# Reordering sums and convolution steps, an early split of `w_out2`, new homes for buffers and narrower mean squares in a fused attention and two-FFN kernel

## The chip, the cores and the metric

The kernel runs on one core of a Trainium2 chip. The metric is the device time of one execution in microseconds (us); lower is better.

## The reference

Eight batches of 576 rows go through linear attention with an RMS norm, a gated feed-forward layer with a spatial product, and a second feed-forward layer with a convolution over the sequence. All of it is in fp32.

```python
kv = einsum('bhsd,bhse->bhde', k, v)              # 8 heads of 64
out = einsum('bhsd,bhde->bhse', q, kv)
x = out / sqrt(mean(out * out, -1) + 1e-6) * g_norm   # -> [8, 576, 512]
h = relu(x @ w_in)                                # 512 -> 1024
u, v = h[..., :512], h[..., 512:]
v_n = (v - mean(v)) / sqrt(var(v) + 1e-6)
gated = u * (w_spatial @ v_n + b_spatial)         # 576 x 576 over the sequence
x = gated @ w_out                                 # 512 -> 512
h = relu(x @ w_in2)                               # 512 -> 1024
c = conv_w[0] * h[s-1] + conv_w[1] * h[s] + conv_w[2] * h[s+1]
out = (h * sigmoid(c)) @ w_out2                   # 1024 -> 512
```

## The kernel before

**Splitting.** Every large product takes fp32 values as a high part (rounded to fp32r by a copy on ACT, functions ending in `_hi`) and a low part (value less high part, on DVE or POOL, functions ending in `_lo`). Three matmuls (`PASSES`) make one product.

**First phase.** `w_out @ w_in2` is multiplied out once at the start (`w_product`). Then `body(b, ahead)` runs for b = 0 to 7 on each engine: PE computes key-value product and attention of batch b+1 (`kv_product`, `o_product`, `square_sum`), the v half (`v_product`, five row tiles i) and u half (`u_product`) of the first layer, and `spatial_product`, four column tiles m. ACT evicts (`v_relu`, `u_relu`, `o_copy`), squares, and takes roots. DVE normalises (`v_stats`, `v_normalise`), inverts the RMS root (`mean_square`, `inverse_root`), scales x, splits, and multiplies by the gate (`gate`, L1045). SP stores the gated activations of a batch and four differences of them (`t_block`, L1092, into the tile `t_then_s`) to a DRAM scratch.

**Second phase.** `body2(b, ...)` runs for b = 0 to 7. The product with the combined weight uses seven products in place of eight for a 2x2 blocking (`PRODUCTS`, Strassen's form as Winograd ordered it), for each of four groups g: `in_product` on PE (L614), six matmuls of 288 columns for each of 28 products a batch. They go to PSUM bank n % 8. ACT copies product 0 of each group (`first_copy`, L905, into `x1`), and DVE makes seven sums from it and the banks (`add`, L1172): the 576 columns of two blocks of h, f = g and f = g + 4. Then for each of the eight blocks e, in `F_ORDER`: relu (ACT, L875), first tap (`tap1`, ACT, L881), two more taps (`tap0`, `tap2`, DVE, L1202 and L1208), sigmoid (ACT, L886), times h (`mul`, DVE, L1213), high part (`h_hi`, ACT, L897 or L899), low part (`h_lo`, DVE, L1218 and L1219). `rows_product` (PE, L622) takes block e of it against `wout2` into four banks, 12 matmuls of 512 columns per e. The last 64 rows of two batches share one more pass of 24 matmuls after each odd batch. In between, the operands of batch b+1 are loaded from the scratch and split (`operand_hi`, L862; `operand_lo`, L1121), seven each.

**What sets the order.** Each engine's order is written out by hand and runs strictly in turn; semaphores join them. In `body2` DVE's loop is

```python
                for e in range(FT + 2):
                    g = e + 1
                    if g < GROUPS: sums_a(b, g)
                    if e < FT: tap0(b, e)
                    if g < GROUPS: sums_b(b, g)
                    if e >= 2: h_lo(b, odd, e - 2)
                    if e < FT: tap2(b, e)
                    if g < GROUPS: sums_c(b, g)
                    if 0 <= e - 1 < FT: mul(b, e - 1)
                if ahead: operand_lo(b + 1, k) for the seven k
```

**Between the phases.** `w_out2` (2 MB) is loaded by SP after the spatial weights are split; its eight blocks are split at the end of the last `body` (ACT L869, POOL L385) into `wout2`, which lies over `w_in`. `x1` lies in `t_then_s`, so the first `first_copy` waits until the last differences are in DRAM (`s_To`). In the last `body`, DVE makes all operand low parts before `gate(3)`, and `in_product` n = 2 waits for that gate.

## Time and profile before

| | |
|---|---|
| three runs | 841.52 us median (839.79 to 842.79) |
| profiled execution | 841.8 us, span of the trace 840.0 us |
| granted TensorE clock | 0.992 of full speed |
| busy share of the span | PE 96%, PE weight load 84%, DVE 72%, ACT 50%, POOL 5% |
| chain that ended last | PE 71%, DVE 18%, ACT 4%, issue 4%, DMA 2% |
| stages by PE | up to 40.1: start and `w_product`; 40.1 to 416.8: first phase; 416.8 to 835.9: second phase |

Busy shares are means over stages; a PE row counts a matmul's whole passage, and matmuls overlap, so the pitch between starts is what a matmul costs. A body of the second phase is read from the start of its first L614 matmul to that of the next body.

### The profile page before, as it was taken

To read this page: it belongs to the slowest core of one execution; us is meant where nothing else is said; L and a number is where in the kernel's file an instruction comes from. 1 tells how busy PE (TensorE), PEld (TensorE's weight loads), DVE (VectorE), ACT (ScalarE), POOL (GpSimd) and SP (SyncE) were. 2 spreads that over 40 slices of the span, in tenths; PEclk is the share of its full clock that TensorE was granted. 3 is DMA by queue.
4 is the path that set the end of the run, shared out by engine and by line. 5 is a ranking of instruction groups with operands and counts; after the bars stand their busy time and mean duration, and the time that the engine had idled before them with its cause. 6 is when DMAs were issued, how large, how long until landed. Compare 5 with 4: busy or idle time off the path is not lost.

```text
span 840.0 us, 16008 instructions
## 1 busy us (share of the span) xinstructions
PE 802.4 (96%) x5910; PEld 704.0 (84%) x5910; DVE 607.5 (72%) x1254; ACT 418.3 (50%) x753; POOL 41.1 (5%) x44
## 2 busy tenths in 40 slices
PE   8998999999999999999969999999999999999998
PEld 7678899897979899898868897978879797796976
DVE  3876666757665766758869878597885978669782
ACT  4654352526343443524715648456473655646563
POOL 3342000000000000000140000000000000000000
PEclk9999999999999999999979999999999999999999
DMA  9862433426262533331322111121201212102101
GB/s 317 276 238 58 181 115 120 179 75 248 71 253 57 197 105 116 106 92 64 114 85 99 51 35 65 64 99 51 99 22 42 98 50 98 50 13 98 50 1 62
DMA packets 34009, 88.48 MB, mean 105 GB/s; under 512 B 2514, under 2 KB 8882, under 8 KB 30004
## 3 DMA queue, kind: packets, MB, share of 16 engines
q1 hardware_dynamic: 33828, 87.99, 31.0%
q8 instruction: 21, 0.34, 0.2%
q14 instruction: 16, 0.13, 0.1%
q10 hardware_dynamic: 144, 0.01, 0.0%
HBM read 61.92 MB, written 26.08 MB: 105 GB/s over the span
## 4 chain that ended last, share of the span: by engine, by line
PE 71%; DVE 18%; ACT 4%; issue 4%; DMA 2%; SPq 0%; DVEq 0%; ACTq 0%
PE ps L446 23%; PE ps L622 17%; PE ps L614 14%; PE ps L477 11%; DVE h_and_sums L1172 3%; DVE work L1213 3%; DVE work L1208 3%; PE ps L397 2%; DVE v_hg_split L1219 2%; PE ps L413 2%; ACT v_hg_split L897 2%; DMA kv_raw<-kv_rest_dram 1%; PE ps L547 1%; DVE t_then_s L1092 1%; PE ps L425 1%
## 5 line engine op out<-in xcount | busy, mean ns | idle before, releaser
L622 PE MATMUL ps<-w_in_split,v_hg_split 128*128 128x512 f32 x832 | 209.1, 398 | 14.7 <-DVE v_hg_split L1219 13.9
L622 PEld LDWEIGHTS ps<-w_in_split,v_hg_split 128*128 128x128 f32 x832 | 151.8, 188 | 66.0 <-DVE v_hg_split L1219 33.5
L446 PE MATMUL ps<-w_sp_split,v_hg_split 128*128 128x288 f32 x896 | 122.2, 297 | 2.8 <-DVE w_sp_split L1061 2.4
L446 PEld LDWEIGHTS ps<-w_sp_split,v_hg_split 128*128 128x128 f32 x896 | 120.8, 190 | 3.5 <-issue 2.6
L446 PE MATMUL ps<-x_operand_split,w_in_split 128*128 128x288 f32 x768 | 104.3, 296 | 1.5 <-ACT work L704 1.5
L446 PEld LDWEIGHTS ps<-x_operand_split,w_in_split 128*128 128x128 f32 x768 | 102.2, 188 | 3.6 <-ACT work L704 1.9
L477 PE MATMUL ps<-w_in_split,x_operand_split 128*128 128x512 f32 x384 | 93.5, 396 | 0.0
L477 PEld LDWEIGHTS ps<-w_in_split,x_operand_split 128*128 128x128 f32 x384 | 70.4, 188 | 20.9 <-issue 6.1
L1172 DVE TENSOR_TENSOR h_and_sums<-t_then_s,ps 128x288 f32<-128x288 f32 x64 | 28.0, 453 | 62.0 <-PE ps L614 41.5
L1172 DVE TENSOR_TENSOR h_and_sums<-h_and_sums,ps 128x288 f32<-128x288 f32 x160 | 66.2, 449 | 8.2 <-PE ps L614 7.4
L614 PE MATMUL ps<-x_operand_split,w_combined_more 128*128 128x288 f32 x384 | 62.3, 298 | 0.0
L1045 DVE TENSOR_TENSOR work<-ps,work 128x576 f32<-128x576 f32 x32 | 24.0, 753 | 48.5 <-PE ps L446 48.5
L875 ACT ACTIVATE h_and_sums<-h_and_sums 128x576 f32<-128x576 f32 x64 | 43.1, 674 | 28.3 <-DVE h_and_sums L1172 28.3
L614 PEld LDWEIGHTS ps<-x_operand_split,w_combined_more 128*128 128x128 f32 x384 | 55.9, 191 | 0.5
L886 ACT ACTIVATE work<-work 128x576 f32<-128x576 f32 x64 | 43.0, 672 | 19.7 <-DVE work L1208 19.7
L1208 DVE SCALAR_TENSOR_TENSOR work<-h_and_sums,const_cols,work 128x576 f32<-128x576 f32 x64 | 51.9, 811 | 0.0
L1202 DVE SCALAR_TENSOR_TENSOR work<-h_and_sums,const_cols,work 128x576 f32<-128x576 f32 x64 | 51.9, 811 | 0.0
L881 ACT ACTIVATE work<-h_and_sums,const_cols 128x576 f32<-128x576 f32 x64 | 49.8, 778 | 2.1
L1213 DVE TENSOR_TENSOR work<-h_and_sums,work 128x576 f32<-128x576 f32 x64 | 48.0, 750 | 0.0
L899 ACT ACTIVATE v_hg_split<-work 128x576 fp32r<-128x576 f32 x32 | 22.0, 687 | 49.9 <-DVE work L1213 49.9
L1012 DVE BATCH_NORM_STATS2 bn_stats<-work 128x6 f32<-128x512 f32 (+1 forms) x40 | 27.6, 691 | 24.7 <-ACT work L699 18.3
L685 ACT ACTIVATE x_operand_split<-o_x 128x576 fp32r<-128x576 f32 x32 | 22.0, 687 | 47.0 <-DVE o_x L995 44.0
(124 smaller groups left out, 1137.4 us busy)
## 6 DMA issues: line engine op xcount, KB each, us to landing
kv_raw<-kv_main_dram SPq DMA_DIRECT2D x8, 2048.0 KB, 9.7
q_raw<-q_T_dram SPq DMA_DIRECT2D x8, 1152.0 KB, 5.3
operand_scratch<-t_then_s SPq DMA_DIRECT2D x8, 1152.0 KB, 5.3
operand_raw<-operand_scratch SPq DMA_DIRECT2D x8, 1152.0 KB, 5.5
out_dram<-work SPq DMA_DIRECT2D x32, 256.0 KB, 2.2
sq_then_r<-r_scratch SPq DMA_DIRECT2D x14, 576.0 KB, 6.3
operand_scratch<-work SPq DMA_DIRECT2D x24, 288.0 KB, 2.6
operand_more_raw<-operand_scratch SPq DMA_DIRECT2D x8, 864.0 KB, 7.2
```

Of the source, the lines that this page charges most:

```text
L446: last = pe.matmul(pair[bank][:, c, :], st, mo[:, c * HALF:(c + 1) * HALF], start=(n == 0), stop=(n == len(steps) - 1))
L477: last = pe.matmul(dst, x, w, start=(n == 0), stop=(n == len(st) - 1))
L614: last = pe.matmul(PS[:, n % 8, 0:HALF], st, mo, start=(i == 0), stop=(i == len(steps) - 1))
L622: last = pe.matmul(PS[:, ROW_BANK[i], :], x, wout2[:, w, F_ORDER[e], :], start=(e == 0 and n == 0), stop=(e == FT - 1 and n == len(PASSES) ...
L875: act.activation(h_sb[f][:, 1:S + 1], h_sb[f][:, 1:S + 1], ACT.Relu).then_inc(s_hr, 1)
L881: act.activation(t_sb[e % 2], h_sb[f][:, 1:S + 1], ACT.Copy, scale=cols[:, FT + f:FT + f + 1]).then_inc(s_t0, 1)
L886: act.activation(p_sb[e % 2], t_sb[e % 2], ACT.Sigmoid).then_inc(s_sig, 1)
L1012: dve.bn_stats(stats[0:n, :], v_sb[i % 2][0:n, :]).then_inc(s_vst, 1)
L1172: dve.tensor_tensor(dst, x, PS[:, (g * NPROD + k) % 8, 0:HALF], ALU.add).then_inc(s_sum, 1)
L1202: dve.scalar_tensor_tensor(out=t, in0=h_sb[f][:, 0:S], scalar=cols[:, f:f + 1], in1=t, op0=ALU.mult, op1=ALU.add).then_inc(s_cv1, 1)
L1208: dve.scalar_tensor_tensor(out=t, in0=h_sb[f][:, 2:S + 2], scalar=cols[:, 2 * FT + f:2 * FT + f + 1], in1=t, op0=ALU.mult, op1=ALU.add).th ...
L1213: dve.tensor_tensor(p_sb[e % 2], h_sb[F_ORDER[e]][:, 1:S + 1], p_sb[e % 2], ALU.mult).then_inc(s_mul, 1)
```

## The change

1. **Order of products and sums.** `PRODUCTS` is permuted so that block f = g is complete after product 4 of a group; `F_ORDER` takes it first. Sums and convolution steps are written out one by one in `body2` on DVE and ACT. `operand_hi` and `operand_lo` 0 to 2 of the next batch move between the last two `h_hi` and `h_lo`.
2. **`w_out2`.** Loaded in two halves by ACT's own queue in the first-phase bodies 1 and 2 (now unrolled), split there by ACT and POOL, stored to a DRAM scratch from ACT's queue, and loaded in split form by SP after batch 7's u products, four DMAs of 1 MB.
3. **Homes.** `x1`, `t_sb[1]`, `p_sb` and `o_sb` get other places; the three waits for stores move from before the second phase to the first sigmoid and the first output copy. The last four differences go to DVE's first `body2`. In the last `body` low parts 5 and 6 come after `gate(3)`.
4. **Weights.** `A12` and `A22` keep their low part in place; one wait of ACT on DVE goes.
5. **Mean squares.** `head_select` has a column per head, so `square_sum` takes 128 rows at once: 16 matmuls in place of 32, and `ms`, `std`, `r0` have 144 columns in place of 288.

```diff
-PRODUCTS = [(A11, B11), (S2, T2), (A12, B21), (S3, T3), (S1, T1), (A22, T4), (S4, B22)]
+PRODUCTS = [(A11, B11), (S2, T2), (A12, B21), (S1, T1), (S4, B22), (S3, T3), (A22, T4)]
-F_ORDER = [4, 0, 5, 1, 6, 2, 7, 3]
+F_ORDER = [0, 4, 1, 5, 2, 6, 3, 7]
...
+        x1 = [WK[:, S:S + HALF], WK[:, 3328:3328 + HALF]]
-        x1 = [TB[:, M + i * HALF:M + (i + 1) * HALF] for i in (0, 1)]
-        ms, std, r0 = (sb(n, [P, CH, QS]) for n in ("ms", "std", "r0"))
+        ms, std, r0 = (sb(n, [P, QS]) for n in ("ms", "std", "r0"))
...
@ SP, behind load_operands(0)
+            sp.wait_ge(s_wo2_st, 2 * DMA)
+            for h in (0, 1):
+                for c, part in ((LO, 0), (HI, 1)):
+                    sp.dma_start(wout2[:, c, h * MT:(h + 1) * MT, :].bitcast(F32),
+                                 wo2_dram[h, :, part * MT * M:(part + 1) * MT * M].rearrange("p (f n) -> p f n", f=MT)).then_inc(s_wo2_ld, DMA)
             store_gated(B - 1)
...
@ PE, square_sum
-                        for c in range(CH):
-                            r = slice(c * D, (c + 1) * D)
-                            last = pe.matmul(PS[g * 32:(g + 1) * 32, SSQ_BANK + c, 0:QS], sel[r, m, :],
-                                             rB[r, m, g * QS:(g + 1) * QS], start=(m == 0), stop=(m == MT - 1))
+                        last = pe.matmul(PS[g * 32:(g + 1) * 32, SSQ_BANK, 0:QS], sel[:, m, :],
+                                         rB[:, m, g * QS:(g + 1) * QS], start=(m == 0), stop=(m == MT - 1))
...
@ ACT, body, at the end of row tile i
+                    if isinstance(b, int) and b in (1, 2):
+                        if i == 0:
+                            wo2_load(b - 1)
+                        else:
+                            wo2_split(b - 1, i - 1)
...
+            def wo2_split(h, f):
+                act.wait_ge(s_wo2_in, (h + 1) * DMA)
+                act.activation(wo2_hi[:, f, :], wo2_raw[:, f, :], ACT.Copy).then_inc(s_wo2_hi, 1)
...
@ ACT, body2
+                h_hi(b, odd, 5)
+                sigmoid(b, 7)
                 if ahead:
+                    operand_hi(b + 1, 0)
+                    operand_hi(b + 1, 1)
+                h_hi(b, odd, 6)
+                if ahead:
+                    operand_hi(b + 1, 2)
+                h_hi(b, odd, 7)
...
@ DVE, body2, groups 2 and 3 alike, then the rest
+                sum_u2_c11(b, 3)
+                mul(b, 1)
+                sum_u4(b, 3)
+                tap0(b, 3)
+                sum_c12(b, 3)
+                sum_u3(b, 3)
+                h_lo(b, odd, 1)
+                sum_c22(b, 3)
+                sum_c21(b, 3)
+                tap2(b, 3)
+
+                mul(b, 2)
+                for e in range(4, FT):
+                    tap0(b, e)
+                    h_lo(b, odd, e - 2)
+                    tap2(b, e)
+                    mul(b, e - 1)
                 if ahead:
+                    operand_lo(b + 1, 0)
+                h_lo(b, odd, FT - 2)
+                mul(b, FT - 1)
+                if ahead:
+                    operand_lo(b + 1, 1)
+                    operand_lo(b + 1, 2)
+                h_lo(b, odd, FT - 1)
```

**ACT, end of the first `body2`.** Sigmoids are L886 before and L915 now, high parts of h L899 and L926, operand high parts L862 and L891, output copies L925 and L988. Before:

```order
L886 ACTIVATE work<-work 128x576
L899 ACTIVATE v_hg_split<-work 128x576
L886 ACTIVATE work<-work 128x576
L899 ACTIVATE v_hg_split<-work 128x576
L862 ACTIVATE x_operand_split<-operand_raw 128x576 x4
L862 ACTIVATE operand_more_split<-operand_more_raw 128x576 x3
L925 ACTIVATE work<-ps 128x512 x4
```

Now:

```order
L926 ACTIVATE v_hg_split<-work 128x576
L915 ACTIVATE work<-work 128x576
L891 ACTIVATE x_operand_split<-operand_raw 128x576 x2
L926 ACTIVATE v_hg_split<-work 128x576
L891 ACTIVATE x_operand_split<-operand_raw 128x576
L926 ACTIVATE v_hg_split<-work 128x576
L891 ACTIVATE operand_more_split<-operand_more_raw 128x576 x2
```

Two operand splits stand ahead of the seventh high part of h, a third ahead of the eighth.

**DVE, end of the first `body2`, now.** L1278 and L1284 are taps, L1289 `mul`, L1294 and L1295 `h_lo`, L1193 `operand_lo`; before, all seven operand splits stood behind the last `h_lo`.

```order
L1284 SCALAR_TENSOR_TENSOR work<-h_and_sums,const_cols,work 128x576
L1289 TENSOR_TENSOR work<-h_and_sums,work 128x576
L1193 TENSOR_TENSOR x_operand_split<-operand_raw,x_operand_split 128x576
L1294 TENSOR_TENSOR rest_split<-work,v_hg_split 128x64
L1295 TENSOR_TENSOR v_hg_split<-work,v_hg_split 128x512
L1289 TENSOR_TENSOR work<-h_and_sums,work 128x576
L1193 TENSOR_TENSOR x_operand_split<-operand_raw,x_operand_split 128x576 x2
L1294 TENSOR_TENSOR rest_split<-work,v_hg_split 128x64
L1295 TENSOR_TENSOR v_hg_split<-work,v_hg_split 128x512
```

One low part of an operand now stands ahead of the seventh `h_lo`, two more ahead of the eighth.

**ACT, first-phase `body` 1, row tiles 0 to 2, now** (with the semaphores waited on). L704 is `v_relu`, L719 `v_hi`, L714 `v_root`, L675 and L680 `o_copy` and `square`:

```order
L680 ACTIVATE sq_then_r<-o_x 128x576 [waits s_xm,s_oc]
L792 DMA w_out_raw<-w_out_dram 128x4x512 [waits s_b,s_sp_lo]
L704 ACTIVATE work<-ps 128x512 [waits s_vlo,s_v]
L719 ACTIVATE v_hg_split<-work 128x512 [waits s_vn]
L714 ACTIVATE vsd<-ve 128x1 [waits s_ve]
L796 ACTIVATE v_hg_split<-w_out_raw 128x512 [waits s_wo2_in]
L704 ACTIVATE work<-ps 128x512 [waits s_vlo,s_v]
L675 ACTIVATE o_x<-ps 128x576 [waits s_xr,s_o]
```

L792 and L796 are new; the third `v_relu` and all that follows it stand behind L796's wait for the load that L792 issued three instructions earlier.

## Rows read from the trace of the kernel before

**Rows 1.** What PE waited for: line, releaser, us in total, times, longest

```profile
PE ps L622 <- DVE v_hg_split L1219: 13.9, 16, 1.1
PE ps L614 <- DVE work L1045: 5.0, 1, 5.0
PE ps L614 <- ACT t_then_s L905: 4.3, 1, 4.3
PE ps L446 <- DVE w_sp_split L1061: 2.4, 1, 2.4
```

**Rows 2.** Timeline of PE: start, length, instructions, idle before; second-phase bodies 0, 1, 2

```profile
416.84 0.96 PE L614 MATMUL ps<-x_operand_split,w_combined_more 128*128 128x288 f32 x6
...
477.66 0.95 PE L614 MATMUL ps<-x_operand_split,w_combined_more 128*128 128x288 f32 x6
...
530.67 0.61 PE L622 MATMUL ps<-w_in_split,v_hg_split 128*128 128x512 f32 x2
...
531.36 0.95 PE L614 MATMUL ps<-x_operand_split,w_combined_more 128*128 128x288 f32 x6
...
558.62 20.64 PE L622 MATMUL ps<-w_in_split,v_hg_split 128*128 128x512 f32 x84 [0.72 <-DVE v_hg_split L1219]
579.10 0.95 PE L614 MATMUL ps<-x_operand_split,w_combined_more 128*128 128x288 f32 x6
```

**Rows 3.** Timeline of DVE in second-phase body 2

```profile
551.48 0.82 DVE L1172 TENSOR_TENSOR h_and_sums<-t_then_s,ps 128x288 f32<-128x288 f32 x2 [1.79 <-ACT t_then_s L905]
...
559.21 0.75 DVE L1213 TENSOR_TENSOR work<-h_and_sums,work 128x576 f32<-128x576 f32 x1
...
572.78 0.69 DVE L1219 TENSOR_TENSOR v_hg_split<-work,v_hg_split 128x512 fp32r<-128x512 f32 x1
...
575.02 0.69 DVE L1219 TENSOR_TENSOR v_hg_split<-work,v_hg_split 128x512 fp32r<-128x512 f32 x1
575.63 2.76 DVE L1121 TENSOR_TENSOR x_operand_split<-operand_raw,x_operand_split 128x576 fp32r<-128x576 f32 x4
```

**Rows 4.** Timeline of ACT in second-phase body 2

```profile
574.76 2.39 ACT L862 ACTIVATE x_operand_split<-operand_raw 128x576 fp32r<-128x576 f32 x4
```

**Rows 5.** Costliest groups: count, busy us, mean ns of one, idle before

```profile
L1172 DVE TENSOR_TENSOR h_and_sums<-h_and_sums,ps 128x288 f32<-128x288 f32 x160 | 66.2, 449 | 8.2 <-PE ps L614 7.4
...
L1208 DVE SCALAR_TENSOR_TENSOR work<-h_and_sums,const_cols,work 128x576 f32<-128x576 f32 x64 | 51.9, 811 | 0.0
```

**Rows 6.** Timeline of DVE between the phases

```profile
417.49 5.32 DVE L1121 TENSOR_TENSOR operand_more_split<-operand_more_raw,operand_more_split 128x576 fp32r<-128x576 f32 x3
```

**Rows 7.** Timeline of POOL, the eight low parts of `w_out2`

```profile
415.65 13.55 POOL L385 TENSOR_TENSOR w_in_split<-w_out_raw,w_in_split 128x512 fp32r<-128x512 f32 x8 [345.79 <-ACT w_in_split L869]
```

**Rows 8.** Timeline of ACT in first-phase body 1

```profile
100.44 0.69 ACT L675 ACTIVATE sq_then_r<-o_x 128x576 f32<-128x576 f32 x1
...
104.57 0.60 ACT L699 ACTIVATE work<-ps 128x512 f32<-128x512 f32 x1 [0.69 <-PE ps L477]
```

**Rows 9.** DMA issues: count, KB each, median us from issue to landing

```profile
q_raw<-q_T_dram SPq DMA_DIRECT2D x8, 1152.0 KB, 5.3
```

**Rows 10.** Stretches: us, busy by engine, PE clock, DMA share, GB/s

```profile
102.00:104.00 2.00, 2.00 (x11) 1.65 (x10) 1.45 (x5) 1.17 (x3) 0.00 (x0) 1.00 1.01 410
```

**Rows 11.** Timeline of DVE in the inverse root, bodies 0 and 1

```profile
68.61 1.57 DVE L980 TENSOR_TENSOR std<-std,ms 128x288 f32<-128x288 f32 x1
...
116.00 1.95 DVE L976 RECIPROCAL r<-std 128x288 f32<-128x288 f32 x1 [0.61 <-ACT std L679]
...
118.48 0.46 DVE L980 TENSOR_TENSOR std<-std,ms 128x288 f32<-128x288 f32 x1
```

**Rows 12.** Timeline of PE, first-phase bodies 3 and 4: square sums, key-value products

```profile
204.46 1.24 PE L425 MATMUL ps<-sq_then_r,head_select 64*32 64x144 f32 x64
205.63 12.99 PE L446 MATMUL ps<-x_operand_split,w_in_split 128*128 128x288 f32 x96
...
233.40 2.55 PE L397 MATMUL ps<-kv_raw 128*64 128x64 f32 x80
```

More of the change, by code:

```diff
@@ L297, in _ @@
                 store_gated(b)
-            sp.wait_ge(s_sp_lo, NT)
-            sp.wait_ge(s_b, 1)
-            sp.dma_start(wo2_raw[:, :, :], w_out2.rearrange("(f p) n -> p f n", p=P)).then_inc(s_wo2_in, DMA)
             spread_r(B - 1)
@@ L757, in body @@
                     u_relu(b, 3)
+                    if isinstance(b, int) and b in (1, 2):
+                        wo2_store(b - 1)
                     for m in range(MT):
@@ L852, in _ @@
             body(0, True)
-            with act.Fori(1, B - 1) as b:
+            body(1, True)
+            body(2, True)
+            with act.Fori(3, B - 1) as b:
                 body(b, True)
@@ L885, in sigmoid @@
                 act.wait_ge(s_hlo, b * FT + max(e - 1, 0))
+                if e == 0 and isinstance(b, int) and b == 0:
+                    for s in s_go:
+                        act.wait_ge(s, DMA * B)
+                    act.wait_ge(s_T, 4 * B)
+                    act.wait_ge(s_wo2_st, 2 * DMA)
                 act.activation(p_sb[e % 2], t_sb[e % 2], ACT.Sigmoid).then_inc(s_sig, 1)
@@ L924, in body2 @@
                     act.wait_ge(s_od[i], DMA * b)
+                    if i == 0 and isinstance(b, int) and b == 0:
+                        act.wait_ge(s_To, DMA * B)
                     act.activation(o_sb[i], PS[:, ROW_BANK[i], :], ACT.Copy).then_inc(s_oev, 1)
@@ L937, in _ @@
             act.wait_ge(s_pad, 1)
-            for s in s_go:
-                act.wait_ge(s, DMA * B)
-            act.wait_ge(s_To, DMA * B)
             run(0, False)
@@ L1221, in body2 @@
             def body2(b, odd, ahead):
-                sums_a(b, 0)
-                sums_b(b, 0)
-                sums_c(b, 0)
-                for e in range(FT + 2):
-                    g = e + 1
-                    if g < GROUPS:
-                        sums_a(b, g)
-                    if e < FT:
-                        tap0(b, e)
-                    if g < GROUPS:
-                        sums_b(b, g)
-                    if e >= 2:
-                        h_lo(b, odd, e - 2)
-                    if e < FT:
-                        tap2(b, e)
-                    if g < GROUPS:
-                        sums_c(b, g)
-                    if 0 <= e - 1 < FT:
-                        mul(b, e - 1)
@@ L1241, in body2 @@
-                if ahead:
-                    for k in range(NPROD):
+                first = isinstance(b, int) and b == 0
+                sum_u2_c11(b, 0)
+                if first:
+                    t_a(B - 1)
+                sum_u4(b, 0)
+                sum_c12(b, 0)
+                if first:
+                    t_b(B - 1)
+                sum_u3(b, 0)
+                if first:
+                    t_c(B - 1)
+                sum_c22(b, 0)
+                sum_c21(b, 0)
+                sum_u2_c11(b, 1)
@@ new lines, in body2 @@
+                tap0(b, 0)
+                sum_u4(b, 1)
+                tap2(b, 0)
+                sum_c12(b, 1)
+                sum_u3(b, 1)
+                tap0(b, 1)
+                sum_c22(b, 1)
+                sum_c21(b, 1)
+                tap2(b, 1)
+                sum_u2_c11(b, 2)
+                mul(b, 0)
+                sum_u4(b, 2)
+                tap0(b, 2)
+                sum_c12(b, 2)
+                sum_u3(b, 2)
+                h_lo(b, odd, 0)
+                sum_c22(b, 2)
@@ new lines, in body2 @@
+                sum_c21(b, 2)
+                tap2(b, 2)
+                sum_u2_c11(b, 3)
[14 more added lines that the diff above has]
+                    mul(b, e - 1)
@@ L1243, in body2 @@
+                if ahead:
+                    operand_lo(b + 1, 0)
+                h_lo(b, odd, FT - 2)
+                mul(b, FT - 1)
+                if ahead:
+                    operand_lo(b + 1, 1)
+                    operand_lo(b + 1, 2)
+                h_lo(b, odd, FT - 1)
+                if ahead:
+                    for k in range(3, NPROD):
                         operand_lo(b + 1, k)
```

194 lines of the change are left out of this document (119 added, 75 removed).

## The prediction

> **What bounds the kernel now.** I read the page first: PE is busy 96% of a span of 840.0 us, so only two things can help, less work for PE or fewer of its waits. The waits of PE come next [rows 1]: the largest sum is rows_product waiting for h_lo, two long waits in each second-phase body; then one stop of 5.0 on a gate and one of 4.3 on first_copy, both between the phases; then 2.4 in first-phase body 0. In the timeline of PE [rows 2] second-phase body 2 lasts 579.10 - 531.36 = 47.74 us and body 1, which has the 24 matmuls for rest rows, 531.36 - 477.66 = 53.70. Body 0 lasts 477.66 - 416.84 = 60.82, 13 more than body 2.
>
> What ends body 2 is seen by joining rows of PE and DVE. The 84 matmuls of e = 1 to 7 take 579.10 - 558.62 = 20.48, 0.244 each, where three in a row without a wait go from 530.67 to 531.36, 0.23 each. The seventh h_lo ends at 572.78 + 0.69 = 573.47 [rows 3], 42.11 after the body's start; PE has 24 matmuls left from there and ends 5.63 later. The last h_lo, 575.71, is 3.39 before the end and does not set it. So a second-phase body is as long as DVE and ACT need to bring the seventh h_lo, plus 5.6.
>
> In the first phase the 2.4 in body 0 is the only stop of PE over 1 us that this view has once the bodies run; from body 1 on PE is the bound.
>
> **Part 1: order in body2, bodies 1 to 6.** Up to mul(2), DVE executes exactly the same instructions in both orders: 28 sums, four of each DVE tap, mul and h_lo of e = 0 and 1. Only its waits differ. Before, mul(2) starts at 559.21, 27.85 after the start [rows 3], and the longest wait on the way is 1.79 on ACT's first_copy for group 3. In the new order I walk the same span: group 0 goes with PE and ends 6.2 after the start; 1.2 and 0.4 waiting for the copy and the third product of group 1; 21 sums, eight taps, two mul and two h_lo in a row, 0.37, 0.73, 0.66 and 0.74 apiece, which is a row's duration less 0.08 or so ([rows 5], and mul and h_lo in [rows 3]), since neighbours overlap as the four splits in 2.76 do, 16.3; and now two waits of the 1.79 kind, since the copies of groups 2 and 3 both stand behind a sigmoid that needs the tap just finished, 1.8 and 1.7. Sum 27.7: the same.
>
> From there both orders repeat tap0, h_lo, tap2, mul at one pace, but a relu now stands ahead of the third h_hi on ACT, +0.3. The tail differs more. Two operand splits stand on ACT ahead of the seventh h_hi. Four in a row take 2.39 [rows 4], 0.57 apart, so h_hi(6) comes 1.1 later and h_lo(6) ends 43.5 after the start where it was 42.1. Behind it DVE has mul, two low parts of 0.67 and h_lo(7), which ends at 46.2; 12 matmuls are left there, 2.8. Both ways give 49.1, against 47.74: **+1.35** for each of bodies 1 to 6, which is +8.1. Body 7 has no operands to split: +0.3. The bounds are what rows allow for the two causes: at least 0 if PE's backlog hides the tail, at most +2.0 if both of ACT's terms and a further 0.6 of the low parts fall on the path. So 0 to +12 for the six.
>
> **Part 2: between the phases.** PE reaches the first in_product at 416.84 as before. Before, DVE made seven low parts ahead of gate(3), three of them in 5.32 [rows 6] beside POOL's splits at 415.65 to 429.20 [rows 7]; PE stood 5.0, then 4.3 for the stores in front of x1, and ran slowly behind both. Now POOL is silent here, low parts 5 and 6 come behind the gate, and x1 needs no store. gate(3) is made when the last spatial product ends, about 417.1, done at 417.8; in_product 2 wants it at 418.4. The four differences now stand in DVE's group 0 and move it back by 1.5 net. So body 0 lasts 49.1 + 1.5 = 50.6 against 60.8: **-10.2**. The seven operand splits hide under spatial products. The first sigmoid now carries the waits for stores. SP issues 4 MB of w_out2 ahead of them at about 402; with 2 MB of operands at 410 GB/s [rows 10] that is done by 420, the stores by 424, and the sigmoid comes at 429. The low bound is that nothing but the two stops goes, -9.3 and -3 of slow matmuls at most, -12; the high bound -8, if ACT or DVE is late by two more.
>
> **Part 3: w_out2 in bodies 1 and 2.** ACT issues 1 MB at the end of row tile 0, 101.1, just behind a square [rows 8]. The first split stands ahead of the third v_relu, which ran at 104.57, and behind that come the copies and squares for which PE's last v_product waits. A lone load of 1152 KB takes 5.3 [rows 9], and here the DMA engines are full with SP's loads of keys, values and queries (410 GB/s, share 1.0 [rows 10]). Sharing alike, 1 MB needs 2.5 to start plus 5.2 at half of 410: it lands about 109. ACT stops for 5, the third v_relu goes from 104.6 to 109.6, the fourth square from 108 to 113.5, and PE, which wanted it at 110.2, loses 3.3. The fourth and fifth v_relu lose more behind three further splits, and POOL's four low parts hold DVE. The shorter inverse root, 1.9 less, gives back the end of that chain. I take **+4.0** a body, +8. Bounds: +1.5 each if the load lands in the 5.3 of [rows 9], +5.5 if it lands at 111: 3 to 11 for both.
>
> While POOL split the spatial weights in body 0, one instruction of the inverse root took 1.57 where it takes 0.46 [rows 11]. By the Trainium skill (SBUF — State Buffer, Who interferes with whom) a DVE instruction with two SBUF inputs is blocked for the whole of a GpSimd instruction that reads SBUF. By that rule, the trace agrees. I count about 1 a body for POOL inside the 4.0, since ACT is the later one for most of it; the whole of it is a rival below.
>
> **Part 4: mean squares.** The reciprocal took 1.95 and three products 0.46 for 288 columns [rows 11]; at half the columns about 1.9 goes from each body, hidden where PE has no gap. In body 0 it is on the path of the 2.4 stop [rows 1], of which 1.9 goes, and part of the slow matmuls behind it: **-3**, bounds -1 to -4. At the start PE is busy with w_product until the root is needed: 0. On PE the square sum takes 205.63 - 204.46 = 1.17 a batch [rows 12] and eight tiles side by side become four with half the matmuls, so I take 0; bounds: half of it gone, -4.7 for all, or twice as long, +9. Key-value products use all 128 rows in two column tiles, and 80 of them pass in 2.5, 0.031 each.
>
> The Trainium skill (TensorE: Matmul & The Clock Gate, The mechanism under Packing small matmuls) says that a weight load overlaps running matmuls only when its row group differs. With all 128 rows no load would be hidden, and the square sum would grow; how far is worked out as a rival below. By that rule, the 0.031 for full-row tiles speaks against it.
>
> **Part 5: the rest.** Weights in place take 2.4 of waits off DVE in the last body; it is inside part 2. Four more memsets lie under the first DMA. Stores of w_out2 from ACT's queue, 2 MB each, come where DMA is idle: 0.
>
> **Sum.** 840.0 + 8.1 + 0.3 - 10.2 + 8.0 - 3.0 = 843.2 in span, +1.8 around it as in the profiled 841.8: 845.0. The median shown is 0.3 below that execution, so **844.6**.
>
> **Rivals.**
> *The tail costs nothing* (0.20). PE's backlog at e = 6 is larger than I think, or the operand halves fit the gaps that DVE had anyway. Then part 1 is +0.3 a body, 844.6 - 6.3 = 838.3, faster than before. For it: 2.24 lie between the last two h_lo [rows 3] where mul and h_lo take 1.4, so 0.8 was free. Against: ACT's two splits stand in front of h_hi(6), not beside it. It decides at an h_lo(6) that ends before 42.5.
> *The load is quick* (0.15): 1.5 a body in part 3, 839.6. For it: descriptors of two queues may not share alike. Against: share 1.0.
> *The body falls to PE's own work* (0.07): 168 matmuls at 12.99/96 = 0.135 [rows 12] and 96 at 0.23 [rows 2], 44.8, which is -2.9 a body. In seven bodies, in place of +8.4: 844.6 - 8.4 - 20.3 = 815.9. For it: DVE has two blocks ready when the products end. Against: its pace per block behind that is unchanged.
> *The first sigmoid waits* (0.11), slower. SP's 6 MB go at two thirds of 410 GB/s, end near 427, the 2 MB of stores behind them near 434; the sigmoid wants them at 429, and DVE's mul and PE follow it, +5: 850. It decides from 429 on.
> *POOL's splits fall on the path whole* (0.05), eight of 13.55/8 = 1.69 [rows 7], +13.5 in place of +8: 850.1. The rule above gives this one. *The square sum doubles* (0.03), +1.17 in each of eight batches: 854.0, the other rule's.
> *The change does not free the stop between the phases* (0.04), another wait takes its place: 854.8.
>
> **Numbers.** The forecast has 0.35. A measurement tells 0.3%, 2.5 us, from no change: 839.0 to 844.0. Faster: the tail, PE's own work, some of the quick load and of the forecast's lower end, 0.32. Slower: the last four rivals and six tenths of the forecast, 0.44. The rest 0.24. The range holds the forecast with its bounds (837 to 851 alone), the tail and the quick load together (833) and the late sigmoid: 833 to 851.
>
> **What would show it.** Right: second-phase bodies of 49 and 55 us by the start of L614; body 0 near 50.6 with no stop of PE before in_product 9; in bodies 1 and 2 a wait of ACT for DMA of 4 to 5, and a first-phase body near 51; body 0 three shorter. Wrong: second-phase bodies below 47.7, L425 rows longer than 1.2, no wait of ACT on w_out_raw, or a wait of the first sigmoid for the scratch.

## The result, and the profile after

The changed kernel takes 856.67 us (median of 4, 855.42 to 857.69) against 841.39 us (839.79 to 842.79) for the kernel before beside it: 1.0182 times the time, 95% interval 1.0158 to 1.0205. Slower was forecast, with 0.44, but by 3; it is 15.3, outside the range. The profiled execution has a span of 853.6 against 840.0, at the same granted clock of 0.992.

First the waits of PE in the changed kernel (us in total, times, longest), to be held against [rows 1]:

```profile
PE ps L627 <- DVE v_hg_split L1295: 17.4, 18, 1.3
PE ps L482 <- ACT work L704: 10.5, 2, 7.4
PE ps L627 <- DVE h_and_sums L1244: 5.5, 7, 1.1
...
PE ps L404 <- DMA kv_raw<-kv_rest_dram: 2.6, 1, 2.6
PE ps L430 <- DVE sq_then_r L1022: 1.7, 1, 1.7
PE ps L451 <- DVE w_sp_split L1121: 1.3, 1, 1.3
```

The stops of 5.0 and 4.3 between the phases are gone. New in second place is `v_product` waiting for ACT's `v_relu` (L704), 10.5 in two waits, and this is in the bodies that carry `w_out2`. The timeline of PE gives the bodies their lengths. First phase, bodies 0 to 2 (start, length, instructions, idle before):

```profile
58.53 1.19 PE L430 MATMUL ps<-sq_then_r,head_select 128*32 128x144 f32 x32
...
74.84 15.08 PE L451 MATMUL ps<-w_sp_split,v_hg_split 128*128 128x288 f32 x112 [1.28 <-DVE w_sp_split L1121]
...
113.61 3.83 PE L482 MATMUL ps<-w_in_split,rest_split 128*128 128x512 f32 x8 [7.41 <-ACT work L704]
...
147.62 2.55 PE L404 MATMUL ps<-kv_raw 128*64 128x64 f32 x80
...
167.12 2.29 PE L482 MATMUL ps<-w_in_split,rest_split 128*128 128x512 f32 x7 [3.10 <-ACT work L704]
```

Second phase, the starts of bodies 0, 1, 2 and 3, with the stops inside body 2; [rows 2] are their counterpart:

```profile
431.83 0.96 PE L619 MATMUL ps<-x_operand_split,w_combined_more 128*128 128x288 f32 x6
...
482.62 0.95 PE L619 MATMUL ps<-x_operand_split,w_combined_more 128*128 128x288 f32 x6
...
537.58 0.95 PE L619 MATMUL ps<-x_operand_split,w_combined_more 128*128 128x288 f32 x6
...
560.93 6.17 PE L627 MATMUL ps<-w_in_split,v_hg_split 128*128 128x512 f32 x24 [0.80 <-DVE h_and_sums L1244]
568.27 11.95 PE L627 MATMUL ps<-w_in_split,v_hg_split 128*128 128x512 f32 x48 [1.17 <-DVE v_hg_split L1295]
581.23 5.76 PE L627 MATMUL ps<-w_in_split,v_hg_split 128*128 128x512 f32 x24 [1.01 <-DVE v_hg_split L1295]
586.83 0.96 PE L619 MATMUL ps<-x_operand_split,w_combined_more 128*128 128x288 f32 x6
```

Body by body, each the difference of two such starts (before's are from its own timeline, read alike):

| us | before | forecast | after | difference |
|---|---|---|---|---|
| first phase, body 0 | 52.1 | 49.1 | 49.4 | -2.7 |
| body 1 | 47.1 | 51.1 | 57.8 | +10.7 |
| body 2 | 47.1 | 51.1 | 54.2 | +7.1 |
| second phase, body 0 | 60.8 | 50.6 | 50.8 | -10.0 |
| bodies 1 to 6, each | 53.7, 47.7 | 55.0, 49.1 | 55.0, 49.25 | +1.3 to +1.5 |

With six of the last kind (+8.4), 0.3 more in the start, 0.2 more in the last body and 0.5 less in the first phase's other five, that is 13.6, the whole difference of the spans. (The profiled execution took 855.4, 1.2 under its median, and that of the kernel before 841.8, 0.4 over its own: that is the way from 13.6 to 15.3.) All lines but two are within 0.3 of the forecast. First-phase bodies 1 and 2 cost 17.8 where 8 stood.

What ACT did there (timeline of ACT, then the DMA issues between 94 and 116 us: count, KB each, us from issue to landing):

```profile
98.13 0.39 ACTq L792 DMA_DIRECT2D w_out_raw<-w_out_dram  x1
...
101.27 0.20 ACT L714 ACTIVATE vsd<-ve 128x1 f32<-128x1 f32 x1 [0.71 <-DVE ve L1077]
112.45 0.63 ACT L796 ACTIVATE v_hg_split<-w_out_raw 128x512 fp32r<-128x512 f32 x1 [10.97 <-DMA w_out_raw<-w_out_dram]
112.98 0.58 ACT L704 ACTIVATE work<-ps 128x512 f32<-128x512 f32 x1
```
```profile
kv_raw<-kv_main_dram SPq DMA_DIRECT2D x1, 2048.0 KB, 11.6
...
q_raw<-q_T_dram SPq DMA_DIRECT2D x1, 1152.0 KB, 8.6
w_out_raw<-w_out_dram ACTq DMA_DIRECT2D x1, 1024.0 KB, 14.3
kv_raw<-kv_rest_dram SPq DMA_DIRECT2D x1, 256.0 KB, 12.9
```

ACT stood for 11.0 in front of the first split, with the third `v_relu` behind it. The load took 14.3 to land. SP had issued the store of 1.2 MB of differences at 93.94 and 2.4 MB of keys and values at 94.91 and 95.77; `w_out2` came behind them at 98.13, and 1.2 MB of queries at 103.45. By issue time plus landing the keys and values were in at 106.5 and 108.7, the queries at 112.1 and `w_out2` last, at 112.4. In body 2 the order was another: issued at 155.90, `w_out2` landed at 165.9, the queries only at 168.7. For body 1 the stretches say the same (us, busy of PE, PEld, DVE, ACT and POOL, PE clock, DMA share, GB/s):

```profile
104.00:106.00 2.00, 2.00 (x10) 1.49 (x8) 0.00 (x0) 0.00 (x0) 0.00 (x0) 1.00 1.03 320
106.00:108.00 2.00, 0.20 (x1) 0.00 (x0) 0.00 (x0) 0.00 (x0) 0.00 (x0) 1.00 1.08 356
108.00:110.00 2.00, 0.00 (x0) 0.00 (x0) 0.00 (x0) 0.00 (x0) 0.00 (x0) 1.00 1.04 432
110.00:112.00 2.00, 0.00 (x0) 0.00 (x0) 0.00 (x0) 0.00 (x0) 0.00 (x0) 0.60 0.27 111
112.00:114.00 2.00, 0.39 (x1) 0.39 (x2) 0.41 (x1) 1.55 (x3) 0.85 (x1) 0.50 0.00 0
```

The DMA engines are full until 110, from 106.2 no compute engine works, and then PE's clock falls to 0.5, the lower of its two levels (1.2 and 2.4 GHz). So the eight matmuls behind the stop take 3.83.

### The profile page after: what moved, and what is told of

Its sections match the earlier page's. It is cut to its first block and busy times, and to the rows that moved or that the text cites. A ratio compares the mean times of both kernels' runs of the same rounds, so it can differ in the third digit from the quotient of the medians.

```text
span 853.6 us, 15487 instructions
## 1 busy us (share of the span) xinstructions
PE 802.4 (94%) x5654; PEld 700.6 (82%) x5654; DVE 588.0 (69%) x1254; ACT 419.3 (49%) x753; POOL 40.1 (5%) x48
## 5 line engine op out<-in xcount | busy, mean ns | idle before, releaser
L451 PE MATMUL ps<-w_sp_split,v_hg_split 128*128 128x288 f32 x896 | 120.4, 295 | 1.7 <-DVE w_sp_split L1121 1.3
L915 ACT ACTIVATE work<-work 128x576 f32<-128x576 f32 x64 | 44.0, 687 | 94.0 <-DVE work L1284 94.0
L1244 DVE TENSOR_TENSOR h_and_sums<-work,ps 128x288 f32<-128x288 f32 x64 | 27.5, 453 | 71.7 <-PE ps L619 39.4
L1105 DVE TENSOR_TENSOR work<-ps,work 128x576 f32<-128x576 f32 x32 | 24.1, 755 | 61.2 <-PE ps L451 61.0
L899 ACT ACTIVATE h_and_sums<-h_and_sums 128x576 f32<-128x576 f32 x64 | 43.1, 674 | 27.9 <-DVE h_and_sums L1244 27.7
L1278 DVE SCALAR_TENSOR_TENSOR work<-h_and_sums,const_cols,work 128x576 f32<-128x576 f32 x64 | 51.9, 811 | 0.0
L1284 DVE SCALAR_TENSOR_TENSOR work<-h_and_sums,const_cols,work 128x576 f32<-128x576 f32 x64 | 51.9, 811 | 0.0
L905 ACT ACTIVATE work<-h_and_sums,const_cols 128x576 f32<-128x576 f32 x64 | 49.1, 767 | 0.5
L1289 DVE TENSOR_TENSOR work<-h_and_sums,work 128x576 f32<-128x576 f32 x64 | 48.1, 751 | 0.0
L1295 DVE TENSOR_TENSOR v_hg_split<-work,v_hg_split 128x512 fp32r<-128x512 f32 x64 | 43.8, 684 | 0.0
## 6 DMA issues: line engine op xcount, KB each, us to landing
w_out_split_scratch<-v_hg_split ACTq DMA_DIRECT2D x2, 2048.0 KB, 10.5
```

The lines of the kernel that those rows point to most:

```text
L451: last = pe.matmul(pair[bank][:, c, :], st, mo[:, c * HALF:(c + 1) * HALF], start=(n == 0), stop=(n == len(steps) - 1))
L899: act.activation(h_sb[f][:, 1:S + 1], h_sb[f][:, 1:S + 1], ACT.Relu).then_inc(s_hr, 1)
L905: act.activation(t_sb[e % 2], h_sb[f][:, 1:S + 1], ACT.Copy, scale=cols[:, FT + f:FT + f + 1]).then_inc(s_t0, 1)
L915: act.activation(p_sb[e % 2], t_sb[e % 2], ACT.Sigmoid).then_inc(s_sig, 1)
L1244: dve.tensor_tensor(dst, x, PS[:, (g * NPROD + k) % 8, 0:HALF], ALU.add).then_inc(s_sum, 1)
L1278: dve.scalar_tensor_tensor(out=t, in0=h_sb[f][:, 0:S], scalar=cols[:, f:f + 1], in1=t, op0=ALU.mult, op1=ALU.add).then_inc(s_cv1, 1)
```

## The experiments

Two theories for bodies 1 and 2: ACT's stand for the load is the cost (1), or the added work itself, four splits on ACT, POOL's hold on DVE and 1 MB more of DMA, is (2). And for the second phase: which part of the new order costs the 1.35 a body, and whether it gives anything. All times are medians beside runs of the kernel before on the same chip (841.52, 841.80 and 841.93 in the three sets). PE's first wait for keys and values, near 16 us, takes 0.9 to 2.6 in different executions, so that spans scatter by over 1 us; body lengths do not, and are compared below.

| run | time | ratio to before (95%) | bodies 1, 2 | body 0 of second phase | odd, even body |
|---|---|---|---|---|---|
| before | 841.5 | | 47.1, 47.1 | 60.8 | 53.7, 47.7 |
| changed | 856.7 | 1.018 (1.016 to 1.021) | 57.8, 54.2 | 50.8 | 55.0, 49.25 |
| e1 split late | 837.2 | 0.995 (0.994 to 0.997) | 47.0, 47.1 | 50.9 | 55.0, 49.25 |
| e2 load early | 838.4 | 0.996 (0.995 to 0.998) | 47.6, 47.6 | 50.8 | 55.0, 49.3 |
| e3 old tail | 847.6 | 1.007 (1.005 to 1.010) | 57.7, 53.6 | 49.7 | 53.9, 48.2 |
| e4 rows of 8 KB | 850.6 | 1.011 (1.009 to 1.013) | 54.8, 53.0 | 50.8 | 55.0, 49.3 |
| e5 mean squares alone | 838.1 | 0.996 (0.994 to 0.997) | 47.0, 47.0 | 60.9 | 53.7, 47.7 |
| e6 low parts first | 854.6 | 1.015 (1.013 to 1.017) | 57.7, 54.8 | 50.0 | 55.0, 49.3 |
| e7 copies first | 828.1 | 0.984 (0.981 to 0.986) | 57.7, 54.3 | 47.3 | 51.8, 45.9 |
| e8 = e1 + e7 | 810.7 | 0.963 (0.961 to 0.965) | 47.0, 47.1 | 47.3 | 51.8, 45.9 |
| e10 = e1 + e3 + e6 + e7 | 802.2 | 0.954 (0.951 to 0.957) | 47.0, 47.2 | 45.4 | 50.7, 44.8 |
| e11 before, copy first | 833.6 | 0.991 (0.988 to 0.993) | 47.1, 47.1 | 61.3 | 52.8, 46.8 |

### e1: the splits of w_out2 at the end of the body

```diff
-                    if isinstance(b, int) and b in (1, 2):
-                        if i == 0:
-                            wo2_load(b - 1)
-                        else:
-                            wo2_split(b - 1, i - 1)
+                    if isinstance(b, int) and b in (1, 2) and i == 0:
+                        wo2_load(b - 1)
...
-                    if isinstance(b, int) and b in (1, 2):
-                        wo2_store(b - 1)
                     for m in range(MT):
                         x_hi(b + 1, m)
+                    if isinstance(b, int) and b in (1, 2):
+                        for f in range(MT):
+                            wo2_split(b - 1, f)
+                        wo2_store(b - 1)
```

> The changed kernel with its load of w_out2 where it is (after row tile 0 of bodies 1 and 2), but with ACT's four splits and the store moved behind the four x_hi at the body's end, when the load has long landed. Bodies 1 and 2 last 57.8 and 54.2 in the changed kernel, 47.05 without w_out2. Theory 1 (the cost is ACT standing for the load, 11.0 and 6.6, with PE starved and slow behind it): both bodies at 47.1 to 48.5, the span shorter by 15 to 18, time about 840. Theory 2 (the cost is the work itself: four splits on ACT, four low parts on POOL that hold DVE, 1 MB beside the other loads): the work is all still there, so at least half of the 17.8 stays, both bodies 50 to 53, time 848 to 854.

Measured: 837.16, 19.5 less than the changed kernel. Bodies 1 and 2 take 47.0 and 47.1 where they took 57.8 and 54.2, 17.8 less: all that the two bodies had cost. The same load, eight splits, POOL's eight low parts and the two stores are still there. In e1's timeline ACT does the four splits in one piece, without a wait, and the eight matmuls that took 3.83 take half of that:

```profile
105.11 1.97 PE L482 MATMUL ps<-w_in_split,rest_split 128*128 128x512 f32 x8
```
```profile
129.54 2.18 ACT L795 ACTIVATE v_hg_split<-w_out_raw 128x512 fp32r<-128x512 f32 x4
```

The load lands no sooner here: the median of the two is 15.8, longer than the 12.2 in the changed kernel. Nobody waits for it. Theory 2 falls.

### e2: the loads a body earlier

```diff
-                        if i == 0:
-                            wo2_load(b - 1)
-                        else:
+                        if i:
                             wo2_split(b - 1, i - 1)
...
                     for m in range(MT):
                         x_hi(b + 1, m)
+                    if isinstance(b, int) and b in (0, 1):
+                        wo2_load(b)
```

> The changed kernel with the splits where they are, between the row tiles, but each load issued a body earlier: behind the four x_hi of bodies 0 and 1 (the second waits there for the store of the first half). Theory 1: the load has landed by the first split, so the stop of 11.0 and 6.6 is gone; left are four splits of 0.6 in ACT's chain and POOL's low parts, both bodies 47.5 to 49.5, time 841 to 844. Theory 2: the splits in the chain and POOL's hold on DVE are the cost: both bodies 51 or more, time 849 or more. If ACT's wait for the store at the end of body 1 holds up its keys and values copy for body 2, body 2 alone stays long by some us.

Measured: 838.35, bodies 1 and 2 both 47.6. The splits are in the middle of ACT's chain, as in the changed kernel, but do not wait (timeline of ACT, load and first split of body 1; DMA issues):

```profile
84.11 0.39 ACTq L792 DMA_DIRECT2D w_out_raw<-w_out_dram  x1
...
101.55 0.62 ACT L796 ACTIVATE v_hg_split<-w_out_raw 128x512 fp32r<-128x512 f32 x1
```
```profile
w_out_raw<-w_out_dram ACTq DMA_DIRECT2D x2, 1024.0 KB, 5.7
```

Issued where SP's large loads are not under way, the same 1 MB lands in 5.7. Splits and POOL's share together cost 0.6 a body; the prediction's 4.0 had held 1 for POOL alone.

### e4: larger pieces for the same load

The host lays `w_out2` out as `[2, 128, 4 * 512]`, so that a partition reads 8 KB in one piece and not four rows of 2 KB. Nothing else differs.

> The changed kernel with w_out2 laid out in DRAM so that each partition's part of a half is 8 KB in one piece instead of four rows of 2 KB. In the changed kernel the two loads land 14.3 and 10.0 after their issue. If the load is slow because its packets are small, it lands in 8 or less and bodies 1 and 2 are shorter by 8 or more. If it is slow because the DMA engines are full with SP's loads of keys, values and queries (share 1.0 until 110) and share in some other way than alike, landing stays at 10 to 14 and the time within 2.

Measured: 850.56, between the two expectations. In body 1 the load lands 10.7 after its issue in place of 14.3, in body 2 9.5 in place of 10.0, and the bodies are 3.0 and 1.2 shorter. The queues between 94 and 116 us, first of the changed kernel, then of e4 (packets, MB, share of 16 engines; q10 is ACT's queue, q1 SP's):

```profile
q1 hardware_dynamic: 1088, 4.72, 57.9%
q10 hardware_dynamic: 528, 1.05, 15.0%
```
```profile
q1 hardware_dynamic: 1058, 4.65, 58.7%
q10 hardware_dynamic: 144, 1.05, 11.5%
```

In body 1, 1.05 MB in 14.3 us are 73 GB/s, a fifth of the 360 or so that moved; in e4 98 GB/s, a quarter. In body 2 it is 105 GB/s, and 110 in e4. So the size of a piece has some part in the share (2.0 KB a packet against 4.3 KB in SP's queue), but even with 7.3 KB ACT's load did not get half. By the Trainium skill (DMA: Bandwidth & Descriptors, Queues, rings and completion order) a DMA engine takes the queues that have work in turn, a packet at a time. The runs agree in so far as larger pieces got more in body 1. The page's packet holds several descriptors, though, while the rows above count 512 packets of 2 KB or 128 of 8 KB and 16 others for one load, so that no share follows from the rule here. What sets the fifth stays open.

### e3: operand splits behind the last h_hi and h_lo

```diff
                 sigmoid(b, 7)
-                if ahead:
-                    operand_hi(b + 1, 0)
-                    operand_hi(b + 1, 1)
                 h_hi(b, odd, 6)
-                if ahead:
-                    operand_hi(b + 1, 2)
                 h_hi(b, odd, 7)
                 if ahead:
-                    for k in range(3, NPROD):
+                    for k in range(NPROD):
                         operand_hi(b + 1, k)
```
DVE's `operand_lo` likewise, behind `h_lo(7)`.

> The changed kernel with the seven operand splits of bodies of the second phase all behind h_hi(7) on ACT and h_lo(7) on DVE, as before the change. Theory 1 (two operand splits ahead of h_hi(6) make h_lo(6) late by 1.1 to 1.4, which sets when the last 24 matmuls of out_product start): an even body 49.25 becomes 48.1, all seven bodies together 7 to 8 shorter, time about 849. Theory 2 (the rest of the order, two waits of 1.8 and 1.7 for the first copies of groups 2 and 3, sets the end alone, and the tail is hidden): no change, within 2. Theory 3: with all splits at the end, the next body's products wait for operands 0 to 2: PE stops up to 1.5 at each start and the time is the same or longer.

Measured: 847.63. Each of the seven bodies with operands ahead is 1.03 to 1.14 shorter, 7.5 in all; the rest of the 9.0 lies ahead of the second phase, in the scatter and bodies 1 and 2. So 1.1 of the 1.3 to 1.5 that each of bodies 1 to 6 lost is the tail, by the path that the prediction gave: two operand splits on ACT in front of h_hi(6).

### e7: the first copies ahead of the sigmoids

```diff
                 h_relu(b, 2)
+                first_copy(b, 2)
                 sigmoid(b, 1)
                 tap1(b, 2)
-                first_copy(b, 2)
...
+                first_copy(b, 3)
                 sigmoid(b, 2)
                 h_relu(b, 4)
-                first_copy(b, 3)
```

> The changed kernel with ACT's first_copy(2) ahead of sigmoid(1) and first_copy(3) ahead of sigmoid(2), in each body of the second phase. DVE's two waits of 1.80 and 1.71 for these copies go. Theory 1 (these waits stand on the chain to h_lo(6), which starts the last 24 matmuls): h_lo(6) ends up to 3.5 earlier, PE's stops of 1.2 and 1.0 in out_product go, and an even body 49.25 falls to what PE itself needs, 22.4 + 6.2 + 12.0 + 5.8 = 46.3; time 834 to 840. Theory 2 (DVE only waits elsewhere, since each sum waits for its product anyway, and the tail of operand splits sets the end): below 1 a body, time 850 or more.

Measured: 828.14, 28.5 less than the changed kernel and 13.4 less than the kernel before, from two moved lines. In the changed kernel DVE stood in front of the sums of groups 2 and 3 in each body (timeline of DVE, body 2):

```profile
552.76 0.82 DVE L1244 TENSOR_TENSOR h_and_sums<-work,ps 128x288 f32<-128x288 f32 x2 [1.80 <-ACT work L932]
...
559.98 0.82 DVE L1244 TENSOR_TENSOR h_and_sums<-work,ps 128x288 f32<-128x288 f32 x2 [1.71 <-ACT work L932]
```

ACT's `first_copy` (L932) stood behind a sigmoid, and the sigmoid needs the tap that DVE makes just ahead of these sums: each engine waited for the other in turn. With the copies first both waits are gone, and all eight bodies are 3.1 to 3.5 shorter: nearly all of the two waits was on the path. PE's stops in body 2 fall to one:

```profile
552.95 16.87 PE L627 MATMUL ps<-w_in_split,v_hg_split 128*128 128x512 f32 x72
570.84 5.75 PE L627 MATMUL ps<-w_in_split,v_hg_split 128*128 128x512 f32 x24 [1.01 <-DVE v_hg_split L1295]
```

### e5: the mean squares in the kernel before

The fifth part of the change alone, in the kernel before: `sel`, `selT`, `square_sum`, `ms`, `std` and `r0` as the change has them.

> The kernel before with one part of the change alone: mean squares in 144 columns (one tile of four mean squares by two halves instead of two, and half as wide ms, std and r). Theory 1: the inverse root is 1.9 shorter and only body 0 has a stop that it ends (2.41), so body 0 goes from 52.1 to 49.4 as in the changed kernel, and all else stays: 2.7 less, time 838.7. Theory 2: body 0 of the changed kernel is shorter for another reason: no change. On PE the square sums stay at 1.12 to 1.2 a batch; twice that would cost 9.

Measured: 838.11, 3.7 less than before. Body 0 of the first phase takes 49.4 as in the changed kernel, 2.7 less; no other body moves by over 0.1, and the rest lies ahead of body 0, in the scatter. Of the 2.7, 1.1 is the shorter stop and 1.5 that 112 matmuls behind it run at full pace:

```profile
73.80 15.09 PE L444 MATMUL ps<-w_sp_split,v_hg_split 128*128 128x288 f32 x112 [1.26 <-DVE w_sp_split L1059]
```

Before, they took 16.61 behind a stop of 2.4. But e11 below, which changes nothing in the first phase, has the same stop and full pace behind it (before, then e11):

```profile
75.66 16.61 PE L446 MATMUL ps<-w_sp_split,v_hg_split 128*128 128x288 f32 x112 [2.41 <-DVE w_sp_split L1061]
```
```profile
75.10 15.09 PE L446 MATMUL ps<-w_sp_split,v_hg_split 128*128 128x288 f32 x112 [2.40 <-DVE w_sp_split L1063]
```

The granted clock from 76 to 80 us was 0.61 and 0.54 before and 1.00 in e11. So the stop of 2.4 is followed by slow matmuls in some executions and not in others. The 1.1 is shown; that the narrower mean squares also saved the 1.5 is not. The median of e5 is 3.7 lower and its times lie closer together (838.0 to 838.9, before 839.9 to 843.6), which fits slow stretches that have become rare, but one trace each doesn't prove it.

### e6: low parts 5 and 6 ahead of the gate again

```diff
-                    operand_lo(0, 3)
-                    operand_lo(0, 4)
+                    for k in range(3, NPROD):
+                        operand_lo(0, k)
                 gate(b, 3)
...
-                else:
-                    operand_lo(0, 5)
-                    operand_lo(0, 6)
```

> The changed kernel with low parts 5 and 6 of the first operands ahead of gate(3) again in the last body of the first phase, as before the change; the splits of w_out2 stay in bodies 1 and 2. The kernel before had stops of 5.0 and 4.3 there. Theory 1 (POOL's splits, which slowed three low parts to 5.32, made the stop): the low parts take 0.7 apiece, gate(3) is at most 1.4 later than now, time within 1.5. Theory 2 (the order alone, low parts ahead of the gate): in_product stops for 3 or more again, time 3 or more longer.

Measured: 854.64, and body 0 of the second phase 50.0 in place of 50.8. No stop came back. In the timeline of DVE the low parts end as `gate(3)` (L1105) can start, at 431.95 here (432.10 in the changed kernel):

```profile
429.14 1.42 DVE L1190 TENSOR_TENSOR operand_more_split<-operand_more_raw,operand_more_split 128x576 fp32r<-128x576 f32 x2
430.48 0.75 DVE L1190 TENSOR_TENSOR x_operand_split<-operand_raw,x_operand_split 128x576 fp32r<-128x576 f32 x1
431.14 0.75 DVE L1190 TENSOR_TENSOR operand_more_split<-operand_more_raw,operand_more_split 128x576 fp32r<-128x576 f32 x1
431.95 0.76 DVE L1105 TENSOR_TENSOR work<-ps,work 128x576 f32<-128x576 f32 x1
```

So the order of low parts and gate alone makes no stop, and moving two low parts behind the gate, into DVE's way at the first sums, cost 0.8. What is left for the stop of 5.0 are two things, and no run takes them apart. Beside POOL's splits three low parts took 5.32 [rows 6], and with the one ahead of them (second line below, before) these four took 6.6, where they take 2.8 here: 3.8 of the 5.0. And DVE came to them later: its third gate (first line) stood 1.3 ahead of the first `in_product` [rows 2] and stands 3.2 ahead of it in e6, since two waits for ACT's high parts of the weights, 1.2 each, are gone.

```profile
415.55 0.75 DVE L1045 TENSOR_TENSOR work<-ps,work 128x576 f32<-128x576 f32 x1
416.22 1.35 DVE L1121 TENSOR_TENSOR x_operand_split<-operand_raw,x_operand_split 128x576 fp32r<-128x576 f32 x1
```

By these figures moving `w_out2` out of this place was the larger part. The other stop, 4.3 for the stores in front of `x1`, is gone in the changed kernel, but no run undoes its part alone.

### e8, e10 and e11: together, and the copy alone in the kernel before

e8 is e1 with e7. e10 adds e3 and e6. e11 is the kernel before with `first_copy(3)` ahead of `h_hi(0)` and `sigmoid(1)`, and nothing else.

> The changed kernel with the splits of w_out2 at the end of bodies 1 and 2 and the first copies of groups 2 and 3 ahead of the sigmoids, both. If both theories hold and act in different places, the gains add: 16 to 18 in bodies 1 and 2 and 17 to 22 in the second phase, time 818 to 824, below the kernel before (841.4). If one of them fails, 835 to 842.

> Four edits to the changed kernel together: splits of w_out2 at the end of bodies 1 and 2, the first copies of groups 2 and 3 ahead of the sigmoids, all operand splits behind the last h_hi and h_lo, low parts 3 to 6 ahead of gate(3). The first two together gave 810.7 with an even body of the second phase of 45.9 and one stop of 1.0 to 1.1 left in each, ahead of the last matmuls, where h_lo(6) comes late behind an operand split. Theory 1 (that stop is the tail's): it goes, even bodies fall to 45.0 and odd ones to 50.9, 6 less, and low parts first give 0.8: time 803 to 806. Theory 2 (the tail is now hidden and splits at the end make the next body's first products wait): 808 to 813.

> The kernel before with one edit: the first copy of group 3 ahead of h_hi(0) and sigmoid(1) on ACT in each body of the second phase; nothing of the change. DVE waited 1.79 for that copy, PE stopped 1.0 and 0.7 behind. Theory 1 (the copy behind a sigmoid is what keeps a body above PE's own work, in either order, and the alternation of sums and steps is itself worth nothing): an even body 47.7 falls to about 46.0, all eight 12 to 14 less, time 828 to 830. Theory 2 (only the new order, with its earlier sums, can use the early copy): less than 4 gained, time 838 or more.

Measured: e8 810.68, 7 below its range; the two gains add. Apart they gave 19.5 and 28.5, together 46.0, and the bodies have the same lengths as alone. The range had been added up from smaller gains. e10 802.23, 0.954 of the kernel before (0.951 to 0.957), faster than both kernels: 39.7 less than before in its own set. PE no longer stops in an even body at all:

```profile
532.34 22.57 PE L627 MATMUL ps<-w_in_split,v_hg_split 128*128 128x512 f32 x96
554.76 0.96 PE L619 MATMUL ps<-x_operand_split,w_combined_more 128*128 128x288 f32 x6
```

That body lasts 44.81: 28 products at 0.80 and 96 matmuls at 0.234, PE's own work.

e11 lies between its theories: 833.64, an even body 46.8 and not 46.0. The bodies of the second phase give 6.1 of its 8.2 in span; 1.5 is the full pace in first-phase body 0, which its edit doesn't touch. The wait of 1.79 went, but PE still stops once and takes the other 84 matmuls in 20.47 from start to start, 0.244 each as before [rows 2], not 0.234:

```profile
551.48 3.00 PE L622 MATMUL ps<-w_in_split,v_hg_split 128*128 128x512 f32 x12
555.18 20.63 PE L622 MATMUL ps<-w_in_split,v_hg_split 128*128 128x512 f32 x84 [0.70 <-DVE v_hg_split L1221]
```

It goes at DVE's pace: `h_lo` starts come 2.98 apart there, and 12 matmuls need 2.8. So the new order of sums and steps is worth something: with copies early and the tail as before in both, 46.8 in the old order against 44.8 in the new, 2.0 a body. With two waits for copies and operand splits in the tail it became a loss of 1.3 to 1.5.

## Why the prediction was wrong

**Part 1, right.** An even body was forecast at 49.1 and takes 49.25, an odd one 55.0 and takes 55.0. The steps hold too: `mul(2)` starts at 565.40, 27.8 after the start (forecast 27.7); DVE waits 1.80 and 1.71 for the copies (1.8 and 1.7); h_lo(6) ends 43.6 after the start (43.5). e3 gives the tail 1.08 and leaves 0.4 for the rest (1.1 and 0.3 forecast). What the text didn't do is ask what the body would be without the two waits that it had worked out. e7 brings it to 45.9 and e10 to 44.8, the figure of the rival *the body falls to PE's own work*.

**Part 2, right.** 50.8 against 50.6, no stop at the start, and a stop of 1.1 at the sums that the four differences delay. Of the causes that it named, low parts 5 and 6 behind the gate were not needed: e6 shows 0.8 the other way. POOL's splits, argued from [rows 6] and [rows 7], fit 3.8 of the stop of 5.0, and the 2.4 of waits for weights of part 5 fit the rest; e6 leaves only these two, and no run undoes either alone. The first sigmoid did not wait for the stores; that rival falls.

**Part 3, the step that failed.** "Sharing alike, 1 MB needs 2.5 to start plus 5.2 at half of 410: it lands about 109." That is 7.9 after its issue; it was 14.3 in body 1 and 10.0 in body 2, and ACT stood 11.0 and 6.7, not 5. In body 1 the load got a fifth of the traffic and not half, and came through with the last of SP's. All of it together, 5.8 MB with the store ahead, ends at 108 by the 410 of [rows 10], which is 9.9 after the issue (98.1 in this trace, 101.1 in the prediction's time) and so the prediction's own high bound. By the 348 that the stretches from 94 to 110 show in the mean, known only afterwards, it ends at 110.5. The second omission is the clock. In body 1 the 10.7 is 8.5 of stops (3.3 forecast) and 1.9 of eight matmuls at half pace. In body 2, where the load landed at that high bound (+5.5), it costs 7.1: 3.9 of stops, nearly as forecast, and 3.2 of slow matmuls, square sums and u products behind them (13.97 for 96 of these in place of 12.98), with a granted clock of 0.50 to 0.69 from 168 to 176 us. About 5 of the 17.8 are thus PE running slowly, for which the prediction had no term. And what it did count, splits and POOL's hold, costs 0.6 a body (e2), or nothing at the body's end (e1).

The rule of the Trainium skill (SBUF — State Buffer, Who interferes with whom) holds in the records. Beside a subtraction on POOL of 1.28 one product of the inverse root takes 0.93 where 0.31 is usual, and a small operation 0.83 for 0.16:

```profile
120.18 0.83 DVE L1090 TENSOR_TENSOR vrs<-vr,vrf 128x1 f32<-128x1 f32 x1 [0.19 <-DVE vrf L1088]
...
125.92 0.93 DVE L1038 TENSOR_TENSOR std<-r 128x144 f32<-128x144 f32 x1
```

The rival drawn from it, all of POOL's time on the path, falls all the same: ACT was the later one.

**Part 4, right in number, in part by luck.** Body 0 is 2.7 shorter against 3, alone (e5) and in the change. The stop shrank by 1.1, not 1.9; the other 1.5 is slow matmuls of the kernel before, which e11 doesn't have behind the same stop. The square sum takes 58.53 to 59.65, 1.12 in place of 1.17, where the rival had it doubled. By itself this doesn't settle the rule of the Trainium skill (TensorE: Matmul & The Clock Gate, The mechanism), a weight load hidden only behind another row group: half the matmuls were saved, and loads that are no longer hidden could have used that up. The same holds for the 0.031 of the prediction. The large matmuls speak against it more plainly. All have 128 rows and a weight load each, and in e10 they start 0.1333 apart with 288 columns and 0.2335 with 512. That is 0.00045 for each further column, by which 288 columns are 0.129: about 0.004 is left for the load, which thus is hidden though the row group is the same. The measurement decides.

**The sum.** Of the 15.3, 3.2 had been forecast and 9.8 is the error of part 3. The other lines of the table add 0.6, and 1.7 is how the profiled executions stand to their medians. The range allowed part 3 11 at most, and it took 17.8; that alone puts the time over 851.

## What to carry to other kernels

Before putting an instruction that waits for a DMA into the middle of an engine's chain, count all bytes already queued and about to be queued on every queue, and take as the high bound that this load lands with the last of them, at a rate below the best that the rows show. Issue it a stage earlier or use its data a stage later: here either gave back about 17 us, and the work itself cost next to nothing. And where one engine's small eviction stands behind an operation that needs the other engine's last result, move the eviction ahead: two lines were worth 26 of span, and they decided whether the new order of the second phase, worth 2.0 a body by itself, gained or lost.

## What the runs showed of the hardware that was not expected

- 1 MB on ACT's queue beside full loads on SP's took 14.3 and 10.0 us to land (15.8 as the median of two in e1), and 5.7 where SP's were not under way. With pieces of 8 KB in place of 2 KB it took 10.7 for 14.3, and 9.5 for 10.0.
- After PE had stood for 7.4 us the granted clock was 0.5 and eight matmuls took 3.83 in place of 1.97. Behind the stop of 3.1 in body 2 the next seven took 2.29 where they need about 1.7, and the clock was 0.60, 0.50, 0.50 and 0.69 in the stretches of 2 us from 168 on.
- The same stop of 2.4 was followed by a granted clock of 0.61 and 0.54 in the kernel before and of 1.00 in e11: it cost 1.5 more in one execution than in the other.
- Square sums on 128 rows in tiles of 32 columns cost 0.035 a matmul, weight loads included. Matmuls of 128 rows by 128 columns, each with its own weight load, start 0.1333 apart with 288 columns and 0.2335 with 512.
